# Attention, a gated layer and a mixture layer on one core: outputs scaled after the matmul, normalisation in pieces with its values in PSUM, up weights staged in a block of their own, and units of the first layer in pairs per token half

## What is computed

```python
# attention: batch 2, 8 heads, 768 tokens, head dim 64; gamma per head
for t in range(S):
    state = gamma * state + outer(k[t], v[t])
    y[t] = scale * q[t] @ state
# layer 1 on x = y as (1536 tokens, 512), d_ff 1536
xn = x / sqrt(mean(x * x) + 1e-6) * rms_g
x = (silu(xn @ w_gate) * (xn @ w_val)) @ w_out
# layer 2: 4 experts of 1024, each token weighted by p
p = domain_probs / (domain_probs.sum(-1) + 1e-9)
out = sum(p[:, e:e+1] * (relu(x @ w1[e]) @ w2[e]) for e in range(4))
```

## Time and profile before

| | us |
|---|---|
| median of 3 runs | 944.17 |
| lowest, highest | 944.05, 947.06 |
| the profiled execution | 939.8 |
| its span in the profile | 938.0 |
| PE busy in the span | 861.9 (92%) |
| DVE, ACT, POOL busy | 526.3, 254.6, 391.3 |

### The profile page before, as it was taken

One profiled execution on the slowest core, in us unless ns is written; L12 is line 12 of the kernel. 1 busy time (PEld: TensorE's weight loads), 2 busy tenths in 40 slices (PEclk: granted clock), 3 DMA queues, 4 the chain that ended last, 5 costly groups with the idle time before them and its releaser, 6 DMA issues.

```text
span 938.0 us, 12393 instructions
## 1 busy us (share of the span) xinstructions
PE 861.9 (92%) x4816; PEld 787.9 (84%) x4816; DVE 526.3 (56%) x827; ACT 254.6 (27%) x502; POOL 391.3 (42%) x354
## 2 busy tenths in 40 slices
PE   7775787989998989987999999999999999999998
PEld 6653687989998989976899999999999999999997
DVE  3566745566565656588455454545454545454545
ACT  3447512322221222233222222222222222222221
POOL 4854208354534353528344352445243524452400
PEclk9887889999998999998999999999999999999999
DMA  9610001100100010100010101010101010101003
GB/s 349 236 58 1 0 1 68 46 23 23 46 23 23 23 45 23 46 22 23 23 46 23 45 23 46 23 45 23 46 23 46 23 46 22 46 22 46 23 1 135
DMA packets 12873, 43.55 MB, mean 46 GB/s; under 512 B 1552, under 2 KB 1552, under 8 KB 12816
## 3 DMA queue, kind: packets, MB, share of 16 engines
q1 hardware_dynamic: 12816, 42.77, 13.3%
HBM read 39.62 MB, written 3.15 MB: 46 GB/s over the span
## 4 chain that ended last, share of the span: by engine, by line
PE 81%; DVE 6%; ACT 5%; POOL 3%; issue 3%; DMA 2%; SPq 0%; DVEq 0%
PE bank L462 26%; PE bank L463 25%; PE bank L464 25%; PE bank L443 2%; PE bank L400 1%; DVE x_all L798 1%; DVE x_sum L812 1%; POOL w_lo L301 1%; DVE x_lo L817 1%; DMA w_raw<-wu 1%; DMA ring<-qkv 1%; PE bank L421 1%; POOL w_raw L291 1%; POOL wd_lo L339 1%; PE bank L433 1%
## 5 line engine op out<-in xcount | busy, mean ns | idle before, releaser
L462 PE MATMUL bank<-x_hi,w_hi 128*128 128x384 f32 x784 | 269.6, 344 | 22.4 <-ACT m L666 7.8
L463 PE MATMUL bank<-x_hi,w_lo 128*128 128x384 f32 x784 | 266.6, 340 | 0.0
L464 PE MATMUL bank<-x_lo,w_hi 128*128 128x384 f32 x784 | 266.2, 340 | 0.0
L911 DVE SCALAR_TENSOR_TENSOR out_acc<-bank,p_norm,out_acc 128x512 f32<-128x512 f32 x180 | 134.9, 749 | 130.8 <-PE bank L464 130.8
L291 POOL TENSOR_TENSOR w_raw<-w_raw 128x256 f32<-128x256 f32 x112 | 81.8, 751 | 299.2 <-DMA w_raw<-wu 297.0
L462 PEld LDWEIGHTS bank<-x_hi,w_hi 128*128 128x128 f32 x784 | 150.2, 192 | 34.3 <-ACT m L666 10.3
L463 PEld LDWEIGHTS bank<-x_hi,w_lo 128*128 128x128 f32 x784 | 150.3, 192 | 5.7 <-issue 0.3
L462 PE MATMUL bank<-wd_hi,h_hi 128*128 128x512 f32 x384 | 149.8, 390 | 2.7 <-DVE out_acc L908 2.0
L464 PE MATMUL bank<-wd_lo,h_hi 128*128 128x512 f32 x384 | 151.9, 396 | 0.0
L463 PE MATMUL bank<-wd_hi,h_lo 128*128 128x512 f32 x384 | 151.5, 395 | 0.0
L464 PEld LDWEIGHTS bank<-x_lo,w_hi 128*128 128x128 f32 x784 | 150.0, 191 | 0.0
(11 more groups left out here) (67 smaller groups left out, 936.8 us busy)
## 6 DMA issues: line engine op xcount, KB each, us to landing
w_raw<-wu SPq DMA_DIRECT2D x28, 512.0 KB, 3.4
ring<-qkv SPq DMA_DIRECT2D x24, 512.0 KB, 6.2
wd_raw<-wd SPq DMA_DIRECT2D x22, 512.0 KB, 3.4
out<-out_acc SPq DMA_DIRECT2D x12, 256.0 KB, 2.0
decay_mask<-t_decay_mask SPq DMA_DIRECT2D x1, 512.0 KB, 5.3
q_decay<-t_q_decay SPq DMA_DIRECT2D x1, 256.0 KB, 8.0
small_sb<-small SPq DMA_DIRECT2D x1, 32.0 KB, 7.0
```

The lines of the kernel that those rows point to most:

```text
L462: pe.matmul(dst, s_hi, m_hi, start=first, stop=False, skip_group_check=True)
L463: pe.matmul(dst, s_lo, m_hi, start=False, stop=False, skip_group_check=True)
L464: return pe.matmul(dst, s_hi, m_lo, start=False, stop=last, skip_group_check=True)
L911: nc.vector.scalar_tensor_tensor(out=to, in0=new, scalar=p, in1=to, op0=ALU.mult, op1=ALU.add).then_inc(posted, 1)
```

## The change

- *Decay as a factor of the outputs.* The mask now depends on the row alone, q is used as loaded, and DVE multiplies the whole output by `y_decay` on its way from PSUM to `x_all` (`scale_y`), where ACT copied it. ACT squares from `x_all` (`square`). `scale_q` is gone.
- *Normalisation spread.* `sum_squares` stands directly behind outputs(n). ACT does logarithm and mean (`guess_log`) in one step, exponential and square (`guess_rstd`) in the next. Mean and rstd stay in bank 7; the next sum of squares waits until x is normalised. The fourth sum of squares stands behind M1 of unit 0.
- *x operands.* Every part has its own semaphore; parts are made in the order of the products. For half 0 they are made from step 6 on. For k = 1, 2, 3 POOL makes S3 and S4 and their remainders; DVE keeps S1 and S2.
- *Weights staged.* One `w_raw` of its own; the next load starts when all remainders of the last block are made (`w_ready`, now counted per product), and only `split_w_hi` waits for the last unit of block c-2.
- *Pairs.* Units of layer 1 run (f,0), (f+1,0), (f,1), (f+1,1). Tiles of a pair are spread over the two units behind it, three and five: none, one and two behind M5, M2 and M7 of the first, two, one and two in the second (`FIRST`, `SECOND`; the first and the last pair differ). Layer 2 starts in the same way with blocks 0 and 1, then goes on as before.
- ACT copies M1 of the next unit before it rounds the last hidden value of this one.

The core of the diff:

```diff
-UNITS1 = [(0, 0), (1, 0), (0, 1), (1, 1)] + [(f, j) for f in range(2, F1) for j in range(J)]
+UNITS1 = [(f + v, j) for f in range(0, F1, 2) for j in range(J) for v in range(2)]
...
-UNITS2 = [(f, j) for f in range(F2) for j in range(J)]
+UNITS2 = [(0, 0), (1, 0), (0, 1), (1, 1)] + [(f, j) for f in range(2, F2) for j in range(J)]
...
-SLOTS1, SLOTS2 = 5, 2
+SLOTS1, SLOTS2 = 4, 2
...
+FIRST, SECOND = (0, 1, 2), (2, 1, 2)
+EARLY, LATE = (0, 0, 2), (2, 2, 2)
...
-                sp.dma_start(w_raw[c % 2][:, 4:8, :, :], wu[c]).then_inc(w_in[c % 2], 16)
+                if c >= 1:
+                    sp.wait_ge(w_ready, NP * c)
+                sp.dma_start(w_raw[:, 4:8, :, :], wu[c]).then_inc(w_in, 16)
 
             def load_wd(d):
+                if d == 1:
+                    sp.wait_ge(norm_done, 3)
+                elif d >= 2:
+                    sp.wait_ge(down_done, tiles_before(d - 2))
...
+                if c >= 2:
+                    pool.wait_ge(up_done, NP * (last_unit(c - 2) + 1))
+                nc.gpsimd.tensor_scalar(w_hi[c % 2][:, :, :, :], w_raw[:, 0:7, :, :], 1.0, 1.0,
+                                        ALU.mult, ALU.mult).then_inc(w_hi_ready, 1)
+
+            def split_w_lo(c, first=0, last=NP):
+
                 pool.wait_ge(w_hi_ready, c + 1)
-                w_split_lo(c, 4, 6)
-                w_split_lo(c, 6, 7)
-
-            def split_t_lo(c):
-                w_split_lo(c, 0, 2)
-                w_split_lo(c, 2, 4).then_inc(w_ready, 1)
+                for _, _, _, ws, _ in PRODUCTS[first:last]:
+                    nc.gpsimd.tensor_tensor(w_lo[c % 2][:, WS[ws], :, :], w_raw[:, WS[ws], :, :],
+                                            w_hi[c % 2][:, WS[ws], :, :].bitcast(F32),
+                                            ALU.subtract).then_inc(w_ready, 1)
...
+            def part_lo(k, name):
+                pool.wait_ge(x_hi_ready[name], k + 1)
+                operand_lo(nc.gpsimd, k, name).then_inc(x_ready[name], 1)
+
+            def sum_3(k):
+                if k < 2:
+                    pool.wait_ge(x_normal, 8 * k + 8)
+                else:
+                    pool.wait_ge(posted, T1N * (F1 - J + k - 2) + 6)
+                token_sum(nc.gpsimd, k, "S3").then_inc(sum_ready["S3"], 1)
+
+            def sum_4(k):
+                if k >= 2:
+                    pool.wait_ge(posted, T1N * (F1 - J + k - 2) + 8)
+                pool.wait_ge(x_ready["S2"], k + 1)
+                token_sum(nc.gpsimd, k, "S4").then_inc(sum_ready["S4"], 1)
```

```diff
+            part_lo(2, "A11")
+            sum_3(2)
+            part_lo(2, "A12")
+            sum_4(2)
+            part_lo(2, "S3")
+            part_lo(2, "A22")
+            part_lo(2, "S4")
...
-                pe.wait_ge(y_taken, 2 * SPB * (k + 1))
+                pe.wait_ge(squares_ready, SPB * (k + 1))
                 if k:
-                    pe.wait_ge(norm_read, 2 * k)
+                    pe.wait_ge(x_normal, 4 * k)
...
                 outputs(n)
+                if n >= SPB and n % SPB == 0:
+                    sum_squares(n // SPB - 1)
...
-                    pe.wait_ge(w_ready, c + 1)
-                    if q == 1:
-                        pe.wait_ge(y_taken, 2 * NSTEP)
+                pe.wait_ge(w_ready, NP * c + PLACE[name] + 1)
...
                 product(q, f, j, k, "M1")
+                if q == 0:
+                    sum_squares(3)
                 product(q, f, j, k, "M5")
-                some(0, 1)
+                some(0)
                 product(q, f, j, k, "M6")
                 product(q, f, j, k, "M2")
-                some(1, 2)
+                some(1)
                 product(q, f, j, k, "M7")
-                some(2, 4)
+                some(2)
```

```diff
+            def square(n):
                 j, a, c = n // SPJ, n // SPB % 2, slice(CH * (n % SPB), CH * (n % SPB) + CH)
-                act.wait_ge(y_done, n + 1)
-                y = bank[4 + n % 2][:, :].rearrange("p (r t) -> p r t", r=KT)
-                nc.scalar.activation(x_all[j][:, :, a, c], y, ACT.Copy).then_inc(y_taken, 1)
+                act.wait_ge(y_taken, n + 1)
                 if n >= 2 * SPB and n % SPB == 0:
                     act.wait_ge(norm_done, n // SPB - 1)
-                nc.scalar.activation(squares[n // SPB % 2][:, n % SPB, :, :], y, ACT.Square).then_inc(y_taken, 1)
+                nc.scalar.activation(squares[n // SPB % 2][:, n % SPB, :, :], x_all[j][:, :, a, c],
+                                     ACT.Square).then_inc(squares_ready, 1)
+
+            def guess_log(k):
+                act.wait_ge(norm_done, k + 1)
+                sums = bank[7][:, 0:TB]
+                nc.scalar.activation(guess[:, :], sums, ACT.Ln, scale=1.0 / DM, bias=eps[:, :]).then_inc(guess_ready, 1)
...
+                act.wait_ge(guess_ready, 3 * k + 1)
+                nc.scalar.activation(guess[:, :], guess[:, :], ACT.Exp, scale=-0.5).then_inc(guess_ready, 1)
+                act.wait_ge(guess_ready, 3 * k + 2)
+                nc.scalar.activation(guess_sq[:, :], guess[:, :], ACT.Square).then_inc(guess_ready, 1)
...
             def unit1(q):
-                copy_up(q, "M1", m1)
+
                 copy_up(q, "M6", u2)
                 sigmoid(q, 0)
                 copy_up(q, "M7", u3)
                 sigmoid(q, 1)
                 hidden_hi(q, 1)
+                if q + 1 < Q1:
+                    copy_up(q + 1, "M1", m1)
                 hidden_hi(q, 0)
...
                 if n >= SPB and n % SPB == 0:
+                    guess_log(n // SPB - 1)
+                if n >= SPB and n % SPB == 1:
                     guess_rstd(n // SPB - 1)
```

```diff
+            def scale_y(n):
+                j, a, c = n // SPJ, n // SPB % 2, slice(CH * (n % SPB), CH * (n % SPB) + CH)
+                dve.wait_ge(y_done, n + 1)
+                nc.vector.tensor_tensor(x_all[j][:, :, a, c], bank[4 + n % 2][:, :].rearrange("p (r t) -> p r t", r=KT),
+                                        y_decay[:, :].rearrange("p (r t) -> p r t", r=KT), ALU.mult).then_inc(y_taken, 1)
+
             def normalise(k):
-                i, j, a = k % 2, k // 2, k % 2
-                dve.wait_ge(guess_ready, 2 * k + 2)
-                nc.vector.scalar_tensor_tensor(out=rstd[:, i, :], in0=rstd[:, i, :], scalar=-0.5, in1=mean_sq[:, i, :],
+                j, a = k // 2, k % 2
+                mean = bank[7][:, 0:TB]
+                dve.wait_ge(mean_ready, k + 1)
+                dve.wait_ge(guess_ready, 3 * k + 3)
+                nc.vector.scalar_tensor_tensor(out=mean, in0=guess_sq[:, :], scalar=-0.5, in1=mean,
                                                op0=ALU.mult, op1=ALU.mult).then_inc(rstd_step, 1)
                 dve.wait_ge(rstd_step, 2 * k + 1)
-                nc.vector.scalar_tensor_tensor(out=rstd[:, i, :], in0=rstd[:, i, :], scalar=1.5, in1=guess[:, i, :],
+                nc.vector.scalar_tensor_tensor(out=mean, in0=mean, scalar=1.5, in1=guess[:, :],
                                                op0=ALU.add, op1=ALU.mult).then_inc(rstd_step, 1)
                 dve.wait_ge(rstd_step, 2 * k + 2)
-                dve.wait_ge(y_taken, 2 * SPB * (k + 1))
                 for r in range(KT):
                     nc.vector.scalar_tensor_tensor(out=x_all[j][:, r, a, :], in0=x_all[j][:, r, a, :],
-                                                   scalar=g_sb[:, r:r + 1], in1=rstd[:, i, :],
+                                                   scalar=g_sb[:, r:r + 1], in1=mean,
                                                    op0=ALU.mult, op1=ALU.mult).then_inc(x_normal, 1)
...
             c22_sum(0)
-            token_sum(1, "S2")
+            normalise(3)
+            sum_of(1, "S1")
+            sum_of(1, "S2")
             gated(0, 0)
-            token_sum(1, "S4")
...
+            unit1(4 * end + 3, (end, 0, 3), (1, 1, 1))
+            sum_of(2, "S1")
+            sum_of(2, "S2")
             post1(end, 0, 6)
             post1(end, 0, 7)
-            token_sum(2, "S3")
             post1(end, 1, 0)
-            token_sum(2, "S2")
+            part_lo(2, "S1")
```

More of the change, by code:

```diff
@@ L388, in _ @@
+            part_lo(3, "S4")
+            split_wd(F1 // 2 + 1)
+            for f in range(2, F2):
                 split_w(F1 + f)
@@ L535, in tile2, with unit1, some @@
                 mm.then_inc(down_done, 1)
-            def unit1(q, k=None, between=None):
+            def unit1(q, k=None, tiles=None, counts=(0, 0, 0)):
                 f, j = UNITS1[q]
-                def some(first, last):
-                    for i in range(first, last):
-                        if between is not None:
-                            tile1(between[0], between[1], 4 * between[2] + i)
+                def some(place):
+                    for i in range(sum(counts[:place]), sum(counts[:place + 1])):
+                        tile1(tiles[0], tiles[1], tiles[2] + i)
@@ L574, in unit2 @@
+            unit1(4 * end + 3, None, (end, 0, 3), (1, 1, 1))
+            for i in range(6, T1N):
```

(36 more changed lines are left out.)

534 lines of the change are left out of this document (218 added, 316 removed).

## The result

The changed kernel takes **899.5 us** in the median of 4 runs (898.21 to 900.48), the kernel before 944.4 us beside it (944.05 to 947.06): a ratio of 0.9518, 95% interval 0.9497 to 0.9539. Its profiled execution took 900.48 us, with a span of 898.7. The forecast was 896, range 880 to 914.

The account below looks back on a forecast made before the run. PE was taken as the bound everywhere but at the beginning. Gains of 20.7 (attention, first units), 27.0 (rest of layer 1) and 1 (layer 2) summed to 48.7 us; with the profile-to-median difference carried over, 896 us, range 880 to 914.

Parts of the forecast that it names:

- Attention and first units: First term, from the start through units 0 and 1: unit 1 ends at 103.0 us, a gain of 20.7 us.
- step 3: Attention, in the walk queue by queue: outputs(3) end at 22.5 us, as before.
- nothing waits for ACT: Attention: ACT does only logarithm and mean before it decays the state, so no queue waits for it.
- PSUM operands: DVE's 24 normalisation instructions, now with one PSUM operand: 0.606 us each, 3.6 us a normalisation, against a median of 1.565.
- Rival 1's rule: DVE in the attention: a VectorE instruction with two SBUF inputs and a GpSimd one exclude each other for a whole instruction.
- rival 1: DVE replaces ACT as the attention's bound; M7 of unit 1 starts some 12 us later: 908 us, chance 0.16.
- Rest of layer 1: Second term, layer 1 from unit 2 on: losses 12.4 us instead of 39.4, a gain of 27.0 us.
- Copy of M1: Layer 1, uncovered unit tails: M6 is late where POOL disturbs DVE's `hid`, 3.3 us lost over five tails.
- The end of the layer: End of layer 1: DVE makes S1 and S2 before it posts tile 6, so PE loses 8.1 us.
- Layer 2: Third term: 510 us against 511.1, a gain of 1 us, with a 4.6 us wait for the second block of weights.
- Rivals 1 and 2: DVE bounds the attention, 908 us, chance 0.16; layer 1's unit tails stay exposed, 909 us, chance 0.08.
- The better case (884): Parts and sums undisturbed, waits at unit 1's M7 and layer 2's second block too short to halve the clock: chance 0.11.

Follow-up runs that it names:

- e12: Changed kernel with each `scale_y` done twice, the first into an unused place: 905.3 us, ratio 0.9584 to the kernel before.
- e8: Changed kernel with a normalisation's exponential taken in its logarithm's step, ahead of the state's decay: 896.2 us, ratio 0.9500 to the kernel before.
- e10: e3 with DVE posting before it sums at layer 1's end, plus e8's edit: 881.8 us, 2.6 us less than without e8's edit side by side.
- e7: Changed kernel with a normalisation's mean and rstd in SBUF instead of PSUM: 905.5 us, ratio 0.9601 to the kernel before.
- e4: Changed kernel with each load of weights held until the last unit of the block before the previous one is done: 898.9 us, ratio 0.9537.
- e5: Changed kernel with a pair's tiles spread evenly again in layer 1, the first one behind M5: 913.3 us, ratio 0.9683 to the kernel before.
- e1: Changed kernel with ACT's rounding of S3, A22, S4 (k=3) moved behind the copies of the second layer-2 unit: 897.8 us, ratio 0.9524.
- e2: Changed kernel with POOL making layer 2's second block of weights ahead of the k=3 parts and the down block: 897.75 us, ratio 0.9521.
- e3: Changed kernel with e1's and e2's moves, and the second down block moved right behind `part_lo(3, "A11")` on POOL: 885.9 us, ratio 0.9398.

## Why the prediction was right, and where it wasn't

The time came out 3.5 us above the forecast, well inside the range, but less by its working than it looks. By spans the gain is 938.0 - 898.7 = 39.3 us, where I had 48.7. By medians it is 44.9, because the profiled execution of before lay 4.6 us under its median and that of after 1 us over. That offset covered over half of an error of 9 us, which is luck.

- **Attention and first units** (20.7, measured 19.3). The walk held step by step: third sum of squares at 54.4, measured 55.97; last one 73.9, 75.63; M7 of unit 1 at 96.5, 97.58, behind 4.6 us and at half clock; unit 1's end 103.0, 104.4. Nearly all of the difference is there at step 3 already (24.25 for 22.5), behind a wait for a DMA of keys. Normalisation instructions are at 0.608 us, and DVE waits for `state_decayed` nowhere. What I took as cost-free was not quite: e12 says that of one more `scale_y` 1.2 of 2.05 us is paid in steps 3 to 5 too, and 5.8 of 8.2 in all. And "nothing waits for ACT" was true of the state alone: e8 shows 3.3 us at the guess (e10 2.6). The reason that I gave for it, that ACT does only logarithm and mean before the decay, holds for a small part: in e8 it does all of it there, and DVE waits for the state 2.4 us in place of 16.3. Of the 19.3 us only the 6.0 of e7 are traced to a cause by a run.
- **PSUM operands** (0.606 taken, against 1.565): right by e7, 6.0 us. The rule of the Trainium skill, "VectorE: DVE Perf Modes", section on the TRN2 errata, by which a PSUM source costs 62 cycles more of fixed time (an estimated 2.3 us over 36 instructions), is not borne out: `x_all` times mean and gain takes 2.19 us for four with `bank` as an operand and 2.20 with `rstd`.
- **Rival 1's rule.** The multiplications slow down only beside POOL and only with both operands in SBUF (5.04 us for four in e7, 2.20 elsewhere). By the Trainium skill, "SBUF — State Buffer", section on the two separate sides, a VectorE instruction with two SBUF inputs and a GpSimd one that reads SBUF exclude each other; e7's slow ones agree. As a bound DVE did not come as far as rival 1 had it.
- **Rest of layer 1** (27.0, measured 27.7; losses 12.4, measured 272.2 - 260.6 = 11.6). No wait for weights came; that the early load has no part in it is shown (e4), that the pairs do it is not. The place of the first tile is worth 13.8 us by e5, where the waits before it showed only 6.1; I had not asked what pairs do to it without that move. Copy of M1: 3.3 taken in five tails, 0.3 found in one. The end of the layer: 8.1 taken, 4.84 of wait and half clock from 365.86 to 370.6 (2.4) found.
- **Layer 2** (gain 1, measured a loss of 7.6). **This is the step that failed:** "the wait for `c` goes ... Late next is the second block of weights." The wait for `w_lo` came as put (4.97 for 4.6), but I walked only POOL's queue to it. The same move, the second block one unit earlier, also put M6 of that unit behind `part_hi(3, "S3")` on ACT, and this behind the same late POOL: 7.47 us and 2.4 of half clock, in no term of the sum. I asked what is queued behind the waiting instruction on PE and on POOL, and not on ACT. The cause is shown by e1, e2 and e3 together: it takes the orders of both queues, POOL's with the down block moved.

Rivals 1 and 2 (908, 909) did not come, though both mechanisms exist at a smaller size. The better case (884) did not come by itself; e3 reaches its figure by another way.

## What to carry to other kernels

When work is moved earlier, walk every queue that feeds it to the new place, and at each instruction that waits ask for the whole chain behind it: where two queues wait for each other, the profile shows one name, and here a fix to either queue alone only moved the wait. So a move that gains nothing alone is no proof against it; try it with its partner. Before a chain is split over steps, undo the split by itself: here the piece that was moved a step later held up what needed its result, and the wait that the split was meant to end had for the most part another cause.
